# A new order of the first half, ScalarE scaling each second expert, and attention in pairs of steps in halves 2, 4 and 6

## The reference, cut to what matters

```python
# 1. linear attention, 8 heads of 48: state decays by w, y = r (state + u k v)
state = wt[:, :, :, None] * state + np.einsum('bhd,bhe->bhde', kt, vt)
# 2. four experts of width 64, the best two of a token weighted by softmax of their logits
scores = softmax(causal(scale * (q @ k.T)));  ye = scores @ v @ wo[e]
out += mask * w[:, :, kk:kk + 1] * ye
# 3. token-shifted mixing: xk, xr = mu * x + (1 - mu) * x_prev
k = np.maximum(xk @ w_k, 0.0);  v = k * k @ w_v;  r = sigmoid(xr @ w_r);  out = r * v
```

## Time and profile before

| | us |
|---|---|
| median of 3 runs | 688.29 (688.19 to 689.12) |
| the profiled execution's own time | 687.9 |
| its span, first to last instruction | 686.2 |
| PE busy | 672.7 (98%) |
| DVE busy | 397.8 (58%) |
| ACT busy | 322.3 (47%) |
| POOL busy | 153.0 (22%) |
| granted TensorE clock, mean | 1.000 |

### The profile page before, as it was taken

One profiled execution on the slowest core, in us unless ns is written; L12 is line 12 of the kernel. 1 busy time (PEld: TensorE's weight loads), 2 busy tenths in 40 slices (PEclk: granted clock), 3 DMA queues, 4 the chain that ended last, 5 costly groups with the idle time before them and its releaser, 6 DMA issues.

```text
span 686.2 us, 12324 instructions
## 1 busy us (share of the span) xinstructions
PE 672.7 (98%) x4800; PEld 443.6 (65%) x4800; DVE 397.8 (58%) x787; ACT 322.3 (47%) x805; POOL 153.0 (22%) x200
## 2 busy tenths in 40 slices
PE   7998999999999999999999999999999999999998
PEld 7876656766657665676656666676665666566554
DVE  7899986292856577546574829647387213561200
ACT  2456656424662266722665237662276323563340
POOL 7663610161203520026010522005320000000000
PEclk9999999999999999999999999999999999999999
DMA  9998500005200170000800053000000000000000
GB/s 237 308 343 229 156 0 1 1 13 161 100 1 1 58 214 2 1 1 25 247 2 1 1 151 122 1 0 2 35 1 0 1 25 12 0 2 12 24 0 34
DMA packets 36921, 43.35 MB, mean 63 GB/s; under 512 B 2560, under 2 KB 27264, under 8 KB 36608
## 3 DMA queue, kind: packets, MB, share of 16 engines
q1 hardware_dynamic: 36864, 42.57, 21.1%
HBM read 37.84 MB, written 4.72 MB: 62 GB/s over the span
## 4 chain that ended last, share of the span: by engine, by line
PE 94%; DVE 3%; POOL 1%; issue 1%; ACT 1%; DVEq 0%; POOLq 0%
PE bank L964 82%; PE bank L968 6%; PE bank L1132 3%; PE bank L1128 3%; DVE idec L683 1%; DVE shared L730 1%; DVE att L753 0%; DVE nmax L717 0%; ACT shared L467 0%; POOL rk_sb L363 0%; ACT shared L476 0%; DVE dec L675 0%; ACT ktok L519 0%; POOL rk_sb L361 0%; POOL state L335 0%
## 5 line engine op out<-in xcount | busy, mean ns | idle before, releaser
L964 PE MATMUL bank<-wv_sb,k_sb 128*128 128x384 f32 x384 | 139.4, 497 | 0.0
L964 PE MATMUL bank<-xk_sb,wk_sb 128*128 128x384 f32 x384 | 136.5, 498 | 0.0
L964 PEld LDWEIGHTS bank<-xk_sb,wk_sb 128*128 128x128 f32 x384 | 68.9, 190 | 44.8 <-issue 5.5
L964 PEld LDWEIGHTS bank<-wv_sb,k_sb 128*128 128x128 f32 x384 | 67.5, 190 | 38.8 <-issue 3.7
L683 DVE RECIPROCAL idec<-dec 112x260 f32<-112x260 f32 x48 | 82.8, 1754 | 0.6
L467 ACT ACTIVATE shared<-bank,nmax 128x128 f32<-128x128 f32 (+5 forms) x96 | 59.9, 630 | 42.3 <-DVE nmax L717 42.3
L394 POOL TENSOR_TENSOR state<-state,carry 112x512 f32<-112x512 f32 x20 | 22.0, 1102 | 247.6 <-DVE state L772 131.1
L964 PE MATMUL bank<-xT_sb,wqk_sb 128*128 128x384 f32 (+1 forms) x240 | 64.1, 424 | 0.6 <-ACT xT_sb L525 0.6
L507 ACT ACTIVATE att<-ident,bonus 128x128 f32<-128x128 f32 x192 | 58.1, 390 | 10.2 <-DVE bonus L691 10.2
L704 DVE TENSOR_TENSOR out_sb<-bank,sg_sb 128x384 f32<-128x384 f32 x24 | 13.4, 557 | 85.2 <-PE bank L964 84.9
L717 DVE TENSOR_REDUCE nmax<-bank 128x1 f32<-128x128 f32 (+5 forms) x96 | 55.4, 618 | 10.0 <-PE bank L964 8.6
(11 more groups left out here) (93 smaller groups left out, 925.5 us busy)
## 6 DMA issues: line engine op xcount, KB each, us to landing
rk_sb<-in_rk SPq DMA_DIRECT2D x24, 384.0 KB, 7.0
v_sb<-in_v SPq DMA_DIRECT2D x24, 256.0 KB, 7.5
w_sb<-in_wT SPq DMA_DIRECT2D x24, 227.5 KB, 5.2
r_sb<-in_rT SPq DMA_DIRECT2D x24, 224.0 KB, 5.1
k_sb<-in_kT SPq DMA_DIRECT2D x24, 224.0 KB, 6.2
out<-out_sb SPq DMA_DIRECT2D x24, 192.0 KB, 1.9
wk_sb<-in_w_k SPq DMA_DIRECT2D x1, 1536.0 KB, 13.1
wv_sb<-in_w_v SPq DMA_DIRECT2D x1, 1536.0 KB, 18.0
```

Source lines behind the costliest of these rows:

```text
L964: return nc.tensor.matmul(out, lhsT, rhs, start=start, stop=stop)
```

## The change

Three things.

**Attention in pairs (halves 2, 4 and 6).** `attention_pair(h, p)` replaces `attention_step`: PE does two score steps, two outputs of the pair before, two hidden groups, two transposes; DVE two maxima, two oT copies, two scales; ACT two exponentials, two relus, two copies, two squares. The transposed probabilities get two sets of blocks and other PSUM banks, the outputs two column ranges of bank 6. The last output moves ahead of the linear steps.

**Less scaling on DVE.** `scale` takes the gate's sum into the 1/sum (one instruction of another kind), and two instructions of `gate_weights` go in every half. In half 0 DVE scales the first expert only and makes a `factor` for the second, which ACT applies in `scale_second`. ACT also makes the first state (`first_state`).

**A new order of half 0** on all engines and of the loads on SP. `decayed` is cut into `hats_by_decay` and `hats_by_inverse`.

```diff
+def pt_bank(h, m, k):
+    if h == 0:
+        return (7, 5)[k]
+    if paired(h):
+        return (4 + m % 2, 2 * (m % 2))[k]
+    return 4 + k
+def paired(h):
+    return 2 <= h < NHF and h % 2 == 0
 def mix_bank(hh, i):
+    if i < FT and paired(hh + 1):
+        return (7, 6, 4, 7, 4, 7, 7, 3)[i]
 # SP
             load_w(0)
+            load_w(1)
+            load_rk(0)
...
+            wqk, wvg, rk(2), w(3), r_k(2), v(1), w(5), v(5), v(3), w(4), r_k(3), r_k(5), r_k(4), v(2), rk(3), v(4), rk(4), rk(5)
 # ScalarE
+            def scale_second(m):
+                w = width(0, m)
+                act.wait_ge(factor_ready, m + 1)
+                a.activation(prob[:, m % 2, w:2 * w], prob[:, m % 2, w:2 * w], ACT.Copy,
+                             scale=factor[:, m:m + 1]).then_inc(prob_scaled_a, 1)
+            keys_by_token(4)
+            scale_second(0)
+            scale_second(1)
             transposed(0, 0)
+            exponentials(0, 2)
+            diagonal(4, 1)
+            scale_second(2)
             first_output(0)
+            exponentials(0, 3)
+            transposed(0, 1)
+            diagonal(5)
+            exponentials(0, 4)
+            first_output(1)
+            transposed(0, 2)
+            scale_second(3)
+            scale_second(4)
+            first_output(2)
+            transposed(0, 3)
+            exponentials(0, 5)
 # VectorE
             def scale(h, m):
-                d.tensor_scalar(rinv[:, two], rsum[:, two], 1e-9, None, ALU.add)
+                d.scalar_tensor_tensor(rinv[:, two], rsum[:, two], 1e-9, bc(gsum...), ALU.add, ALU.mult)
                 d.reciprocal(rinv[:, two], rinv[:, two])
+                if h == 0:
+                    d.tensor_tensor(factor[:, m:m + 1], ...).then_inc(factor_ready, 1)
-                for e in range(2):
+                for e in range(1 if h == 0 else 2):
+            maxima(0, 2)
+            scale(0, 1)
+            state_update(3)
+            maxima(0, 3)
+            bonuses(5)
+            inverse(5, 1)
+            scale(0, 2)
+            maxima(0, 4)
+            masks(4)
+            scale(0, 3)
+            maxima(0, 5)
+            state_update(4)
+            scale(0, 4)
+            scale(0, 5)
+            masks(5)
 # TensorE
+            def attention_pair(h, p):
+                two = (2 * p, 2 * p + 1)
+                if p < HC:
+                    for i in two:
+                        score_step(h, i)
+                    if p >= 1:
+                        for m in two:
+                            output(h, m - 2)
+                for g in two:
+                    for q in range(KT * g, KT * (g + 1)):
+                        mix(h - 1, q)
+                for m in two:
+                    if p < HC:
+                        transposes(h, m)
+                    else:
+                        output(h, m - 2)
-            keep_warm(WARM_UP)
+            keep_warm(18)
+            keep_warm(14)
...
+            score_step(0, 0)
+            x_chunk(3)
+            score_step(0, 1)
+            keys_by_token(4)
+            score_step(0, 2)
+            transposes(0, 0)
+            update(3)
+            score_step(0, 3)
+            transposes(0, 1)
+            output(0, 0)
+            update(4)
+            score_step(0, 4)
+            transposes(0, 2)
+            linear_scores(4)
+            output(0, 1)
+            score_step(0, 5)
+            output(0, 2)
+            transposes(0, 3)
+            linear_scores(5)
+            output(0, 3)
+            transposes(0, 4)
+            x_chunk(4)
+            output(0, 4)
+            transposes(0, 5)
+            x_chunk(5)
+            output(0, 5)
```

More of the change, by code:

```diff
@@ L50 @@
 LAST = NHF - 1
-WARM_UP = 36
 SUM_BANK = (0, 1, 4)
@@ L294, in _ @@
             load_v(0)
-            load_r_k(2)
-            load_rk(2)
-            load_v(1)
             sp.dma_start(wqk_sb[:, :, :], wqk).then_inc(L_QK, 16)
             sp.dma_start(wvg_sb[:, :, :], wvg).then_inc(L_VG, 16)
-            load_v(2)
[L301 to L309, removed]
+            load_rk(2)
+            load_w(3)
+            load_r_k(2)
+            load_v(1)
+            load_w(5)
+            load_v(5)
+            load_v(3)
+            load_w(4)
+            load_r_k(3)
+            load_r_k(5)
+            load_r_k(4)
+            load_v(2)
+            load_rk(3)
+            load_v(4)
+            load_rk(4)
+            load_rk(5)
             sp.dma_start(mu_sb[:, :, :], mu).then_inc(L_MU, 16)
@@ L498, in attention_step @@
                     transposed(h, i - 1)
+            def attention_pair(h, p):
+                two = (2 * p, 2 * p + 1)
+                if p < HC:
+                    for i in two:
+                        exponentials(h, i)
+                for m in two:
+                    relu(h - 1, m)
+                if p < HC:
+                    for m in two:
+                        transposed(h, m)
+                for m in two:
+                    square(h - 1, m)
             def diagonal(n, half=None):
@@ L519, in keys_by_token, with first_state @@
                 a.copy(ktok[:, U % 2, :, :].rearrange("p a r -> p (a r)"), bank[:, 4, 0:PAIRS * R]).then_inc(ktok_ready, 1)
+            def first_state():
+                act.wait_ge(upd_psum, 1)
+                for e in range(2):
+                    new = bank[ROWS[e], 5, :].rearrange("p (a x) -> p a x", a=PAIRS)[:, :, e * HV:(e + 1) * HV]
+                    i = a.copy(state[ROWS[e], 1, :, e, :], new)
+                i.then_inc(state_sum, 1)
             def x_chunk(n):
@@ L909, in _ @@
                 n0 = HC * (h + 1)
-                if h > 0:
+                if paired(h):
+                    for p in range(HC + 1):
+                        attention_pair(h, p)
+                elif h > 0:
                     for i in range(A_STEPS - 1):
@@ L918, in _ @@
                     linear_step(h + 1, s)
-                    if s == 0:
+                    if s == 0 and not paired(h):
                         attention_step(h, A_STEPS - 1)
@@ L933, in _ @@
                 keys(h + 1, 0)
+                if h == 0:
+                    bonuses(NC)
+                    bonuses(NC + 1)
                 if has(h + 2):
@@ L981, in mix @@
                         pe.wait_ge(r_ready, (hh + 1) * HC)
+                    elif hidden and i > 1 and paired(hh + 1):
+                        if i in (3, 5, 6):
+                            pe.wait_ge(relu_ready, hh * FT + (1, 4, 6)[(3, 5, 6).index(i)])
                     elif hidden and i > 0:
@@ L1235, in _ @@
             update(0)
-            keep_warm(4)
             x_chunk(0)
@@ L1281, in _ @@
                     pe.wait_ge(proj_dve, h * (QM + HC))
-                    for i in range(A_STEPS - 1):
-                        attention_step(h, i, True)
+                    if paired(h):
+                        for p in range(HC + 1):
+                            attention_pair(h, p)
+                    else:
+                        for i in range(A_STEPS - 1):
+                            attention_step(h, i, True)
                 if h == LAST:
```

245 lines of the change are left out of this document (149 added, 96 removed).

## The result

| | before | after |
|---|---|---|
| median of 20 runs each | 688.28 (687.54 to 689.13) | 690.34 (687.77 to 693.12) |
| ratio | | 1.0026, interval 1.0016 to 1.0036 |
| granted TensorE clock, mean of each run | 1.000 in all | 0.982 to 0.993 |
| profiled execution: span | 686.2 | 691.4 |
| experts' sum of half 0 starts | 71.07 | 81.87 |

What follows compares the result with a forecast made beforehand. PE was taken to bound the kernel behind half 0, the lists of DVE and ACT within it. Pairs -4.6, their waits +0.3 and half 0 +1.0 gave -3.3: median 685.0 us from 688.3, range 680.5 to 688.2.

Steps and rivals of the forecast that it cites:

- Part 1: Halves 2, 4 and 6: pairs save PE's switches between groups, 1.54 us a half (1.14 to 1.88), 4.6 in all.
- No wait, and no room: First pair of each paired half: the second scale ends near 186.1, PE wants it at 185.93 + 0.2.
- waits of later pairs: Halves 2, 4 and 6: PE waiting for DVE in later pairs, 0.1 us a half, 0.3 in all, bounds 0 and 3.
- rivals 2 and 4: Halves 2, 4, 6: PE waits for scales in every later pair, 691.9, chance 0.07; pairs save nothing, 689.6, chance 0.07.
- Part 2, the walk: Half 0, new lists walked: first score step at 41.8, experts' sum at 72, +1.0 us (bounds -5.5 and +4).
- `keep_warm(4)`, 8 records, goes: 0.85: Half 0 before its first score step: removing these dummy matmuls saves PE 0.85 us.
- Hidden by 1 to 3 us: Half 0 loads: v of chunk 2 lands near 30 to 32 us, PE wants it at about 33.
- its maximum and exponentials 1.1: Half 0: the walk's time between score step 1 and score step 2, 1.1 us.
- Small DVE instructions at 0.2 each: Half 0 walk: each small instruction of DVE, such as those leading to a factor, is taken at 0.2 us.
- each of the four passes through ACT and DVE can be 0.5 to 1 late: +4: Half 0 behind its first score step: upper bound of its change, +4 us, where +1.0 was taken.
- Rival 3: Half 0: PE runs at half rate after idle stretches of 2 and over 3 us; 687 to 689 us, chance 0.11.
- one fall costs about 2 us, two 4: Half 0: price of PE's half rate after idle stretches, read from the first stretch after the idle start.

Runs made afterwards that it cites:

- pairs_gates: Before with attention in pairs in halves 2, 4 and 6 and after's scale and gate arithmetic, half 0 as before; 682.28 us.
- fill_all: After with dummy matmuls in five PE waits of half 0: fill_both's four and 10 ahead of output(0, 3); 687.06 us.
- order_v3_fill: order_v3 with dummy matmuls in PE's waits, 4 ahead of x_chunk(0) and 3 ahead of score step 2; 680.47 us.
- fill_both: After with dummy matmuls in half 0: 4 ahead of x_chunk(0), 3, 5 and 13 ahead of score steps 2, 3 and 4; 687.85 us.
- pairs_second: pairs_gates with ACT scaling each second expert, scale_second(m), right ahead of each transposed(0, m); 693.06 us.
- fill_early: After with only keep_warm(4) put back ahead of x_chunk(0); 690.40 us.
- order_alone: After without its pairs: every half but 0 goes step by step; 695.12 us.
- idle_3: pairs_gates with PE also waiting, ahead of half 0's experts' sum, for a later reciprocal of DVE; 688.94 us.
- order_v3: order_v2 with scale_second(1) on ACT moved behind transposed(0, 0) and exponentials(0, 2); 681.64 us.
- order_v2: scale2_early with scale_second(4) on ACT moved behind first_output(2) and transposed(0, 3); 683.53 us.
- scale2_early: After with scale(0, 2) on DVE moved ahead of maxima(0, 3), bonuses(5) and inverse(5, 1); 684.57 us.

## Why the prediction was wrong

Three terms, each measured by medians against before:

| | forecast | measured | from |
|---|---|---|---|
| pairs and gates | -4.3 | -6.6 | pairs_gates |
| order of half 0, full clock | +1.0 | +5.0 | fill_all less pairs_gates |
| falls of the clock | 0 | +3.7 | after less fill_all |
| sum | -3.3 | +2.1 | |

Two steps failed, the order's term and the clock's. With the order wrong and the clock held the time is fill_all's 687.06, still inside the range; the falls took it out.

**Part 1: right in its mechanism, low in its size.** Switches on PE are what the pairs save: 1.8 us a half, between the 1.54 taken and the upper bound 1.88. The merged score steps gave more than the 0.2 each: the row of 8 matmuls on 256 keys takes 1.06 to the next group, two single ones took 1.38, so 0.32; two of 384 keys 1.49 for 1.70, so 0.21. By its traces pairs_gates saves 1.67 from the first score step to the linear steps, and 1.8 in the half; the rest wasn't followed. "No wait, and no room" was right to the tenth: without the two gate instructions PE waits 0.3. The 0.3 us put down for waits of later pairs did not come; rivals 2 and 4 are out.

**Part 2, the walk: right in where it waits, short in how long.** ACT idles ahead of `scale_second(2)`, released by DVE, and PE idles ahead of score step 4, as forecast. Against the two traces:

| | walk | fill_all | after |
|---|---|---|---|
| score step 0 starts | 41.8 | 43.7 | 45.2 |
| factor 1, ACT goes on | 47.95 | 50.7 | 51.75 |
| score step 4 starts | 55.4 | 58.7 | 59.8 |
| factor 4, ACT goes on | 62.8 | 66.5 | 70.0 |
| experts' sum | 72.0 | 76.3 | 81.9 |

At full clock the walk is 4.3 short.
- *Up to score step 0*, 1.9. "`keep_warm(4)`, 8 records, goes: 0.85", and as much at the start, were counted as gained. But DVE's new list starts `masks(0)` at 16.64, for 15.18 before, and `x_chunk(0)` waits for it: it starts at 18.12 in after and at 18.38 in fill_all, for 18.25 before, where no wait stood ahead of it. So none of the 1.7 arrived. "Hidden by 1 to 3 us" failed too, for v of chunk 2: PE met it 1.22 us early in fill_all, 0.52 in order_v3_fill; two waits of before in this stretch (0.67 and 0.59) are gone in return.
- *The gates*, 0.8 more by factor 1: the leg "its maximum and exponentials 1.1" left DVE's `gate_weights(0, 0)` out, which stands between the two maxima. The two items overlap. In fill_both, with the same lists, score step 0 starts at 42.67, 1.0 earlier than in fill_all, and score step 2 only 0.3 earlier, since it then waits longer for the gates.
- *The rest*, about 1.5 from factor 1 to the end. "Small DVE instructions at 0.2 each" holds some 0.9 of it: in fill_all factor 2 took 0.52 and factor 4 0.71, beside POOL's work. Some 0.4 are the ten dummies of fill_all itself.

So the walk saved time on PE that DVE's new list takes back, left the gates out, and took small DVE instructions from a quieter place than where they stand. The bound "each of the four passes through ACT and DVE can be 0.5 to 1 late: +4" is meant against before, like its lower one of -5.5, and does not hold the +5.0.

**The clock: the step that took it out of the range.** Rival 3 came true, at 0.11. The prediction walked an idle stretch of 3 us and then left the clock out of the forecast's sum, as if the two were separate chances; here they were one, and the term put at 0 measured +3.7. In the table, the ten kernels whose clock reads below 0.999 in most runs have as PE's longest wait in half 0 one of 1.45 to 4.07 us in their profiles; in the others, before among them, it is 0.99 to 1.40. The price "one fall costs about 2 us, two 4" came out near for the two together (3.3 to 3.7), but by luck: it came from a cold start, where the low rate ended within 4 us, while by the medians the early fall cost little or nothing and the late one all of it. In after's profile the late one lasted some 17 us, over a stretch in which PE had no slack left: from score step 4 to the experts' sum it takes 22.1 us for 17.6 in fill_all, 4.5 more; 1.0 was lost ahead of it. The Trainium skill (TensorE: Matmul & The Clock Gate, HAM oscillation) names the mechanism, a wait between bursts that brings the throttled clock back, and the traces agree: behind waits of 3.80 and 4.07 us the granted clock reads 0.50.

**The range** ended at 688.2, just over rival 3's middle. It took the bound of half 0 and the clock's 2 to 4 apart, never together, though the same waits make both. With half 0 at +4 for +1 and two falls, 685.0 + 3 + 4 would have been 692.

## What to carry to other kernels

- An engine that works in order pays for a small job with everything queued behind it. Before a scaling, a copy or a sum is handed to another engine, ask when its input is ready there, and put it behind whatever is ready sooner and ahead of whatever is ready later. Moving three such calls was worth 8.7 us; the work itself was 0.4 to 0.6 us a piece. The same calls behind late exponentials (pairs_second) cost 10.8.
- Where a walk of the lists leaves PE idle for more than a microsecond, the clock belongs in the forecast: here it cost 3 us behind one wait of 4.07 us, and 3.3 to 3.7 in after.
- Merging groups on a PE without slack was a gain in each of the three halves, 1.8 us each. Check that each helper's result is there a few tenths before the merged group wants it.

## What the runs showed of the hardware

**Falls of the granted clock.** In the profiles of after, fill_early, order_alone and idle_3 a fall came with waits of PE of 3.8 and 4.1 us. Shorter waits had one only at some places. Ahead of `x_chunk(0)`, 0.71 us behind another wait: behind 1.24 (after), 1.45 (order_v3), 1.64 (order_alone) and 1.86 us (order_v2) the clock fell, behind 0.96 (scale2_early) and 0.99 us (fill_all) it did not. Ahead of score step 3 one and the same wait, 1.55 us, has a fall behind it in scale2_early and order_v2 and none in after, fill_early and order_alone. So the length of a wait alone does not decide it. Before has a wait of 1.40 us ahead of transposes and reads 1.00. It also varies from execution to execution of one kernel: after's twenty lie 5.4 us apart, before's 1.6, and before too reads 0.998 now and then. What decides it is left open. The low level lasted 6.5 and 17 us in after, some 10 in fill_early and some 7 in idle_3, the last 4.6 of them under work.

**DVE beside POOL.** The factor and scale instructions take longer where POOL has work of its own. POOL's timeline of after and its next activity:

```profile
57.39 0.68 POOL L421 TENSOR_TENSOR k_sb<-k_sb,idec 112x256 f32<-112x256 f32 x1 [9.51 <-DVE idec L791]
58.03 1.05 POOL L444 TENSOR_TENSOR state<-state,carry 112x512 f32<-112x512 f32 x1
68.92 1.05 POOL L444 TENSOR_TENSOR state<-state,carry 112x512 f32<-112x512 f32 x1 [9.85 <-DVE state L903]
```

and DVE's, away from POOL and beside it:

```profile
66.32 0.16 DVE L839 TENSOR_TENSOR factor<-rinv,gate 128x1 f32<-128x1 f32 x1
66.39 0.41 DVE L842 TENSOR_SCALAR shared<-shared,rinv,gate 128x256 f32<-128x256 f32 x1
...
69.27 0.71 DVE L839 TENSOR_TENSOR factor<-rinv,gate 128x1 f32<-128x1 f32 x1
```

The factor takes 0.16 alone and 0.52 and 0.71 beside POOL, the scale of 256 columns 0.41 and 1.22. The Trainium skill (GPSIMD Engine Reference, Specifications) says that the two engines share their interfaces to SBUF, with contention for DVE instructions that have two SBUF inputs or run in a 2-port mode. The factor, with its two inputs, agrees (0.52 and 0.71 for 0.16); the mode of the scale no trace here shows. No run took POOL's work away, so the cause is read from the overlap and not shown by an experiment.
